# A two-network kernel for one core: the lower weight parts of the first network are added up by DMA instead of subtracted on GpSimd

## The chip, the core and the metric

One core of a Trainium2 chip runs the whole program. The metric is the device time of one execution in microseconds, from the first to the last instruction with what the launch puts around it. The core has five engines that run their own instruction streams and meet only at semaphores: TensorE (PE in the profile; its weight loads are PEld), VectorE (DVE), ScalarE (ACT), GpSimd (POOL) and SyncE (SP, which here only issues DMAs). Sixteen DMA engines move the data of every DMA, whoever issued it.

## What is computed

Three stages on 3072 tokens (4 batches of 768) of width 384 (8 heads of 48):

```
# 1. a complex linear recurrence per head
S_re, S_im = ar * S_re - ai * S_im + kv, ar * S_im + ai * S_re
y[t] = q[t] @ S_re
# 2. the first network (384 -> 1536 -> 384)
xn = x / rms(x) * rms_g
x = (silu(xn @ w_gate) * (xn @ w_val)) @ w_out
# 3. the second network (384 -> 2048 -> 384)
return softplus(x @ w_in) @ w_out2
```

All of it is float32. The large products run in TensorE's faster float32r form, in which an operand keeps fewer bits. So that nothing is lost, each weight w is kept as a pair: an upper part (w rounded to float32r) and a lower part (w minus the upper part). Each product is three matrix products: upper times upper, lower times upper, upper times lower.

## The kernel before

The recurrence is cut into 24 units of 128 tokens (NU). For unit n, VectorE and ScalarE turn the decay factors into packed keys and queries `pk`. SyncE stores `pk` to a scratch in DRAM (`rows_scratch`, L347) and loads it back turned to head rows, `mm` (L340, four DMAs, two for each half of the heads). TensorE then does, for unit m = n - 1 and for each half: transposes of the keys (`kt_of`, L1337), scores (`scores`, L1346), and outputs with the state update (`outputs`, L1357 to L1361). Between them VectorE masks the scores (`mask`, L1026), ScalarE copies the turned keys (`kt_copy`, L610) and the outputs (`y_copy`, L616), and VectorE adds to the state (`state_add`, L1032). TensorE's transposes of the second half wait for the `state_add` of the first, and that one waits for `y_copy`.

The first network works on tiles of 512 tokens, four units each. TensorE's work on tile 0 begins when six units have been prepared (LEAD = 6) and all 36 weight blocks of the first network stand in SBUF. So there is a stretch ahead of tile 0 with steps for units 0, 1 and then a loop of four (`Fori(0, LEAD - 2)`), in which the weights are loaded and split: nine blocks of 128x384 in each step, three groups of three (gate, value, out).

A block passes three engines. SyncE loads it into a staging tile, `stage1[:, kind]`, which lies in `ytile` (`load_w1`, L353). ScalarE copies it into an even slot of `slab`, which rounds it (`w1_hi`, L629, counter `w_hi`). GpSimd subtracts the even slot from the staging tile and writes the odd slot (`w1_lo`, L505, counter `w_lo`). There is one staging tile for each kind, so SyncE loads the next block of a kind only when `w_lo` says that the last one was subtracted.

The order of every engine is written out by hand in its `step`. ScalarE's: the first group of `w1_hi` behind `mid_rest`; then the sums of x, the end roots, `kt_copy` of the first half, and the front of unit n + 1 (`front_sq`, L562, which needs `a_in`; `front_ln`, L566, which needs VectorE's `sum_of`, L839; `front_r0`, L570 and L572; `in_time`, L576); then the second group of `w1_hi`; then `y_copy` of the first half; then the third group, `kt_copy` of the second half, `xh_of` (L623) and `y_copy` of the second half. SyncE's: three loads of weights, the loads of v, `mm` (first half), `a_in` (L325), `mm` (second half), `kq_in` (L329), then six more loads of weights, then the store of `pk`.

At the end of the stretch TensorE waits for `w_hi` and `w_lo` (L1447, L1448) and enters the tiles.

Of the kernel before, what the change touches and what calls it, by code (L numbers as in the profile page):

```python
# [18 lines left out]
F32 = mybir.dt.float32  # L19
F32R = mybir.dt.float32r  # L20
I32 = mybir.dt.int32
ALU = mybir.AluOpType
ACT = mybir.ActivationFunctionType
# [12 lines left out]
F1 = 1536 // P  # L36
# [65 lines left out]
def need(eng, sem, value):  # L102

    if isinstance(value, int) and value <= 0:
        return
    eng.wait_ge(sem, value)


def w2_slot(kind, f):

    if f < F1:
        return 6 * f + 2 * kind
    return 6 * (f - F1 + 4 * kind) + 4
# [16 lines left out]
def program(nc, a_d, kq_d, v_d, w1_d, w2_d, g_d, fa_d, fv_d, out_d):  # L130
    ctx = ExitStack()
    with ctx:
        def sb(name, shape, dt=F32):
            return ctx.enter_context(nc.sbuf_tensor(name, shape, dt))
# [4 lines left out]
        def sem(name):  # L139
            return ctx.enter_context(nc.semaphore(name))  # L140
# [9 lines left out]
        slab = sb("slab", [P, 6 * F1, DM], F32R)  # L150
# [72 lines left out]
        ys_done, y_copied, s_added, decayed = [sem(f"ys_done{i}") for i in range(2)], sem("y_copied"), sem("s_added"), sem("decayed")  # L223
        xt_done, xh_done, xl_done = sem("xt_done"), sem("xh_done"), sem("xl_done")
        w_loaded = [sem(f"w_loaded{i}") for i in range(3)]
        w_hi, w_lo = sem("w_hi"), sem("w_lo")
        w2_loaded = [sem(f"w2_loaded{i}") for i in range(3)]
        w2_hi, w2_lo = sem("w2_hi"), sem("w2_lo")
        gv_done, silu_done, p_done = sem("gv_done"), sem("silu_done"), sem("p_done")
# [26 lines left out]
        stage1 = ytile[:, :, :].rearrange("p a b -> p (a b)")[:, 0:3 * DM].rearrange("p (k n) -> p k n", k=3)  # L256
# [59 lines left out]
        def _(sp):  # L316
            def after(*waits):

                for sem_, value in waits:
                    need(sp, sem_, value)  # L320
# [28 lines left out]
            def load_w1(f):  # L349
                for kind in range(3):  # L350

                    after((w_lo, 3 * f + kind + 1))
                    sp.dma_start(stage1[:, kind, :], w1_d[f, kind]).then_inc(w_loaded[kind], 16)  # L353

            def load_w2(slot):
# [111 lines left out]
        @block.gpsimd  # L467
        def _(pool):
            pool.memset(ident[:, :], 0.0).then_inc(const_gp, 1)
            pool.memset(causal[:, :], 1.0).then_inc(const_gp, 1)  # L470
            pool.memset(state[:, :, :], 0.0).then_inc(const_ready, 1)
            pool.memset(zero[:, :], 0.0).then_inc(const_ready, 1)
            pool.memset(half[:, :], 0.5).then_inc(const_ready, 1)
            pool.memset(eps[:, :], 1e-6).then_inc(const_ready, 1)
            pool.memset(one[:, :], 1.0).then_inc(const_ready, 1)
            pool.memset(tiny[:, :], 1e-22).then_inc(const_ready, 1)
            pool.memset(keep[:, :], 1.0).then_inc(const_gp, 1)
            pool.memset(ok[:, :], 1.0).then_inc(const_ready, 1)
            pool.memset(carry[:, :], 1.0).then_inc(const_ready, 1)
            for buf in (ga, gb):  # L480
                pool.memset(buf[:, 0, :, :], 1.0).then_inc(const_ready, 1)
                pool.memset(buf[:, 1, :, :], 0.0).then_inc(const_ready, 1)
            pool.memset(frame[:, 0, :], 1.0).then_inc(const_ready, 1)
            pool.memset(frame[:, 1, :], 0.0).then_inc(const_ready, 1)
            pool.wait_ge(const_gp, 3)
            pool.affine_select(out=ident[:, :], in_=ident[:, :], compare_op=ALU.not_equal, fill=1.0, base=0,
                               pattern=[[-1, P]], channel_multiplier=1).then_inc(const_ready, 1)

            pool.affine_select(out=causal[:, :], in_=causal[:, :], compare_op=ALU.is_ge, fill=0.0, base=0,
                               pattern=[[1, BK], [BK, NBK]], channel_multiplier=-1).then_inc(const_ready, 1)  # L490

            pool.memset(keep[:, 0::UNITS_B], 0.0).then_inc(const_ready, 1)


            pool.sem_inc(w_lo, 3)

            for counter, start in ((xt_done, 1), (xh_done, 1), (xl_done, 1), (silu_done, 1),
                                   (y_stored, 16), (o_stored, 16)):
                pool.sem_inc(counter, start)

            def w1_lo(f):
                for kind in range(3):
                    pool.wait_ge(w_hi, 3 * f + kind + 1)
                    slot = 6 * f + 2 * kind
                    pool.tensor_tensor(slab[:, slot + 1, :], stage1[:, kind, :], slab[:, slot, :].bitcast(F32),  # L505
                                       ALU.subtract).then_inc(w_lo, 1)

            def w2_lo_of(slot):
                q0 = sum(len(x) for x in W2_PLAN[:slot])
                for i, (kind, f) in enumerate(W2_PLAN[slot]):  # L510
                    at_ = w2_slot(kind, f)
                    pool.wait_ge(w2_hi, q0 + i + 1)
                    pool.tensor_tensor(slab[:, at_ + 1, :], stage2[:, i, :], slab[:, at_, :].bitcast(F32),
                                       ALU.subtract).then_inc(w2_lo, 1)

            def lo(T, f):
                pool.wait_ge(hi_done, F1 * T + f + 3)
                pool.tensor_tensor(pl[:, f % 2, :], hid[:, f % 2, :], ph[:, f % 2, :].bitcast(F32),  # L518
                                   ALU.subtract).then_inc(lo_done, 1)

            def tile(T, last=False):
                for i in range(UT):
                    if last and i:
                        w2_lo_of(3 * i - 1)
                    lo(T, 3 * i)
                    if last:
                        w2_lo_of(3 * i)
                    lo(T, 3 * i + 1)
                    if last:
                        w2_lo_of(3 * i + 1)  # L530
                    lo(T, 3 * i + 2)
                if last:
                    w2_lo_of(F1 - 1)

            with pool.Fori(0, F1) as f:
                w1_lo(f)
            with pool.Fori(0, NT - 1) as T:
                tile(T)
            tile(NT - 1, last=True)

            def lo2(T, f):
                pool.wait_ge(hi2_done, F2 * T + f + 1)
                pool.tensor_tensor(pl[:, f % 2, :], hid[:, f % 2, :], ph[:, f % 2, :].bitcast(F32),  # L543
                                   ALU.subtract).then_inc(lo2_done, 1)

            with pool.Fori(0, NT) as T:
                for f in range(F2):
                    lo2(T, f)
# [3 lines left out]
        def _(act):  # L552
# [73 lines left out]
            def w1_hi(f):  # L626
                for kind in range(3):
                    act.wait_ge(w_loaded[kind], 16 * (f + 1))
                    act.activation(slab[:, 6 * f + 2 * kind, :], stage1[:, kind, :], ACT.Copy).then_inc(w_hi, 1)  # L629

            def w2_hi_of(slot):
                q0 = sum(len(x) for x in W2_PLAN[:slot])
                for i, (kind, f) in enumerate(W2_PLAN[slot]):
                    act.wait_ge(w2_loaded[i], 16 * (sum(1 for q in range(q0) if W2_RANK[q] == i) + 1))

                    act.wait_ge(gv_done, 2 * F1 * (NT - 1) + 2 * slot + 2)
                    if slot >= 2:
                        act.wait_ge(out_done, F1 * (NT - 1) + slot - 2 + 3)
                    act.activation(slab[:, w2_slot(kind, f), :], stage2[:, i, :], ACT.Copy).then_inc(w2_hi, 1)
# [12 lines left out]
            def y_out(T):  # L652
                act.wait_ge(out_done, F1 * T + 2)
                act.wait_ge(y_stored, 16 * (T + 1))
                act.wait_ge(w_lo, 3 * F1 + 3)
                for m in range(2):
                    act.activation(ytile[:, m, :], ybank[m][:, :], ACT.Copy).then_inc(y_act, 1)  # L657

            def step(n, m, x, par=0, col=0, T=None, i=0, w1=None, last=False):
# [7 lines left out]
                if w1 is not None:  # L667
                    w1_hi(w1)
# [25 lines left out]
                if w1 is not None:  # L694
                    w1_hi(w1 + 1)
                if m is not None:
                    y_copy(m, 0)
                if T is not None and i == 0:
                    y_out(T)
                if T is not None:  # L700
                    silu(T, 3 * i + 2)
                if w1 is not None:
                    w1_hi(w1 + 2)
# [123 lines left out]
        def _(dve):  # L827
# [242 lines left out]
            def y_out(T):  # L1070
                dve.wait_ge(out_done, F1 * T + 2)
                dve.wait_ge(y_stored, 16 * (T + 1))
                dve.wait_ge(w_lo, 3 * F1 + 3)
                dve.tensor_copy(ytile[:, 2, :], ybank[2][:, :]).then_inc(y_dve, 1)

            def step(n, m, x, par=0, col=0, T=None, i=0):
# [61 lines left out]
                if T is not None and i == 0:  # L1138
                    y_out(T)
# [185 lines left out]
        def _(pe):  # L1325
# [119 lines left out]
            with pe.Fori(0, LEAD - 2) as k:  # L1445
                step(k + 2, k + 1, k)
            pe.wait_ge(w_hi, 3 * F1)  # L1447
            pe.wait_ge(w_lo, 3 * F1 + 3)  # L1448

            for m in range(NJ):  # L1450
                pe.matmul(ybank[m][:, :], slab[:, 0, 0:P], ph[:, 0, :], start=True, stop=False)
# [143 lines left out]
```

## Time and profile before

| | |
|---|---|
| median of 3 runs | 1201.85 us (1201.65 to 1202.08) |
| time of the profiled execution | 1201.7 us |
| span in its profile, first to last instruction | 1199.9 us |
| around the span | 1.8 us |
| TensorE busy | 1078.1 us, 90% |
| VectorE busy | 725.9 us, 60% |
| ScalarE busy | 665.8 us, 55% |
| GpSimd busy | 295.6 us, 25% |
| GpSimd's 36 subtractions of first-network weights (L505) | 37.1 us, 1051 ns each |
| ScalarE's 36 copies of them (L629) | 17.3 us between 56 and 175 us |
| DMA | 91.22 MB |

Busy shares are means over the whole program. The stretch that the change touches lies between 56 and 175 us; from 175 us on the program is in the tiles.

### The profile page before, as it was taken

The numbers are of one execution on the slowest core, as the hardware profiler recorded it, in microseconds if no ns is written. First come the engines' busy times: TensorE is split into PE (matmuls) and PEld (weight loads), VectorE is DVE, ScalarE is ACT, GpSimd is POOL, SyncE is SP. The second block draws the span as 40 slices with busy tenths as digits, with TensorE's granted clock in tenths as the row PEclk, the third lists the DMA queues.
The fourth block names the chain that finished last, engine by engine and source line by source line (L and its number), as shares of the span: only waits on it lengthen the run. The fifth ranks groups of instructions, "written<-read, shape, count | busy, mean of one in ns | idle before, by whom it ended". The sixth has DMA issues, their size and how long they took to land.

```text
span 1199.9 us, 18970 instructions
## 1 busy us (share of the span) xinstructions
PE 1078.1 (90%) x5495; PEld 915.0 (76%) x5495; DVE 725.9 (60%) x2227; ACT 665.8 (55%) x1184; POOL 295.6 (25%) x260
## 2 busy tenths in 40 slices
PE   0555569999999999999999999989999999999996
PEld 0444468888888788888888878868888888888885
DVE  7799988999999899999999411212221213122211
ACT  3344446566655655565655333456676666676663
POOL 0033331111111111111111115643333333333332
PEclk9999999999999899999999999989999999999999
DMA  1455542443343333334432303320010101010000
GB/s 57 112 147 151 142 140 81 122 120 104 87 113 87 89 87 112 107 100 136 115 88 73 100 1 94 113 97 1 1 53 1 53 1 52 0 52 0 26 1 27
DMA packets 63851, 91.22 MB, mean 76 GB/s; under 512 B 4624, under 2 KB 53648, under 8 KB 63760
## 3 DMA queue, kind: packets, MB, share of 16 engines
q1 hardware_dynamic: 63760, 90.15, 26.4%
q8 instruction: 40, 0.66, 0.2%
q14 instruction: 51, 0.42, 0.1%
HBM read 60.89 MB, written 29.24 MB: 75 GB/s over the span
## 4 chain that ended last, share of the span: by engine, by line
PE 32%; issue 32%; DVE 13%; POOL 10%; DMA 6%; ACT 4%; SPq 1%; DVEq 1%; POOLq 0%; ACTq 0%
PE gbank L1329 14%; POOL pl L543 10%; PE ybank L1329 8%; DVE prep L835 5%; DMA rows_scratch<-pk 3%; PE sbank L1346 3%; DMA mm<-rows_scratch 2%; PE xbank L1358 2%; PE xbank L1357 2%; DVE pk L835 2%; PE xbank L1337 1%; PE xbank L1361 1%; ACT front L562 1%; DVE ga L835 1%; DMA a_in<-in_a 1%
## 5 line engine op out<-in xcount | busy, mean ns | idle before, releaser
L1329 PE MATMUL gbank<-xh,slab 128*128 128x512 f32 x1296 | 406.0, 395 | 3.4 <-issue 2.0
L1329 PE MATMUL ybank<-ph,slab 128*128 128x512 f32 x1020 | 319.6, 395 | 4.9 <-ACT ytile L657 4.0
L1329 PEld LDWEIGHTS gbank<-xh,slab 128*128 128x128 f32 x1296 | 242.5, 190 | 52.8 <-issue 2.1
L1329 PE MATMUL gbank<-xl,slab 128*128 128x512 f32 x648 | 254.0, 392 | 0.0
L1329 PEld LDWEIGHTS ybank<-ph,slab 128*128 128x128 f32 x1020 | 189.3, 189 | 43.2 <-issue 5.7
L518 POOL TENSOR_TENSOR pl<-hid,ph 128x512 fp32r<-128x512 f32 x72 | 98.8, 1372 | 467.6 <-ACT ph L650 467.6
L1329 PE MATMUL ybank<-pl,slab 128*128 128x512 f32 x510 | 199.6, 391 | 0.0
L543 POOL TENSOR_TENSOR pl<-hid,ph 128x512 fp32r<-128x512 f32 x96 | 125.7, 1310 | 268.2 <-ACT ph L772 268.2
L1213 DVE SCALAR_TENSOR_TENSOR hid<-gbank,hid 128x512 f32<-128x512 f32 x72 | 49.7, 691 | 214.5 <-ACT hid L763 214.5
L1329 PEld LDWEIGHTS gbank<-xl,slab 128*128 128x128 f32 x648 | 122.5, 189 | 26.3
L1337 PE MATMUL xbank<-ident,mm 96*128 96x96 f32 x192 | 28.3, 277 | 95.3 <-DMA mm<-rows_scratch 74.5
L1329 PEld LDWEIGHTS ybank<-pl,slab 128*128 128x128 f32 x510 | 96.1, 188 | 20.6
L650 ACT ACTIVATE ph<-hid 128x512 fp32r<-128x512 f32 x72 | 45.9, 637 | 106.8 <-PE ybank L1329 101.4
L1337 PEld LDWEIGHTS xbank<-ident,mm 96*128 96x128 f32 x192 | 20.9, 156 | 107.5 <-issue 102.2
L1067 DVE TENSOR_TENSOR hid<-gbank,hid 128x512 f32<-128x512 f32 x72 | 49.4, 686 | 86.2 <-PE gbank L1329 82.1
L772 ACT ACTIVATE ph<-hid 128x512 fp32r<-128x512 f32 x96 | 60.6, 631 | 72.4 <-DVE hid L1213 70.3
L835 DVE TENSOR_TENSOR prep<-prep 128x384 f32<-128x384 f32 (+2 forms) x264 | 89.5, 368 | 1.7
L1357 PE MATMUL xbank<-v_in,at 128*128 128x48 f32 x384 | 80.7, 296 | 5.3 <-issue 3.3
L1358 PE MATMUL xbank<-state,mm 96*128 96x48 f32 x384 | 83.8, 304 | 0.0
L1357 PEld LDWEIGHTS xbank<-v_in,at 128*128 128x128 f32 x384 | 69.0, 220 | 8.4 <-issue 6.9
L763 ACT ACTIVATE hid<-hid,one 128x512 f32<-128x512 f32 x96 | 69.4, 723 | 3.2
L505 POOL TENSOR_TENSOR slab<-ytile,slab 128x384 f32 x36 | 37.1, 1051 | 130.1 <-ACT slab L629 129.9
(126 smaller groups left out, 1597.1 us busy)
## 6 DMA issues: line engine op xcount, KB each, us to landing
rows_scratch<-pk SPq DMA_DIRECT2D x24, 771.0 KB, 4.9
mm<-rows_scratch SPq DMA_DIRECT2D x96, 192.8 KB, 4.0
a_in<-in_a SPq DMA_DIRECT2D x24, 384.0 KB, 4.7
kq_in<-in_kq SPq DMA_DIRECT2D x24, 384.0 KB, 5.8
ytile<-in_w SPq DMA_DIRECT2D x36, 192.0 KB, 4.7
prep<-in_w SPq DMA_DIRECT2D x32, 192.0 KB, 2.5
y_scratch<-ytile SPq DMA_DIRECT2D x7, 768.0 KB, 5.4
v_in<-in_v SPq DMA_DIRECT2D x24, 192.0 KB, 4.5
```

The costliest lines, as they stand in the source:

```text
L518: pool.tensor_tensor(pl[:, f % 2, :], hid[:, f % 2, :], ph[:, f % 2, :].bitcast(F32), ALU.subtract).then_inc(lo_done, 1)
L543: pool.tensor_tensor(pl[:, f % 2, :], hid[:, f % 2, :], ph[:, f % 2, :].bitcast(F32), ALU.subtract).then_inc(lo2_done, 1)
L650: act.activation(ph[:, f % 2, :], hid[:, f % 2, :], ACT.Copy).then_inc(hi_done, 1)
L763: act.activation(hid[:, f % 2, :], hid[:, f % 2, :], ACT.Ln, bias=one[:, 0:1]).then_inc(l_done, 1)
L772: act.activation(ph[:, f % 2, :], hid[:, f % 2, :], ACT.Copy).then_inc(hi2_done, 1)
L835: tick(dve.tensor_tensor(out, a, b, op))
L1067: dve.tensor_tensor(hid[:, f % 2, :], gbank[(2 * f + 1) % 3][:, :], hid[:, f % 2, :], ALU.mult).then_inc(p_done, 1)
L1213: dve.scalar_tensor_tensor(out=hid[:, f % 2, :], in0=hbank[f % 4][:, :], scalar=0.0, in1=hid[:, f % 2, :], op0=ALU.max, op1=ALU.add).then_ ...
L1329: last = pe.matmul(out, slab[:, slot + part, cols], x, start=f, stop=l)
L1337: last = pe.transpose(xbank[:, h * 2 * D:(h + 1) * 2 * D], mm[:, hf * HH + h, 0:CH], ident[0:2 * D, 0:2 * D])
L1357: pe.matmul(xbank[:, h * D:(h + 1) * D], at[:, h, :], v_in[:, head, :], start=True, stop=False)
L1358: pe.matmul(xbank[:, h * D:(h + 1) * D], mm[:, head, CH:2 * CH], state[:, head, :], start=False, stop=True)
```

## The change

ScalarE, having written the upper part into the even slot, waits for its own write and then writes the negative of it into the odd slot (counter `w_neg`). GpSimd no longer computes: it waits for `w_neg` and issues a DMA that reads the block a second time from DRAM and adds it onto the odd slot, which gives w minus the upper part there. Its completion counts on `w_lo`, now by 16 for each block. SyncE's loads and the two `y_out` now wait for `w_neg` in place of `w_lo`, since only ScalarE reads the staging tile. TensorE's entry to the tiles waits for all 36 adding DMAs, and once more on `silu_done`, which has been counted up long before. GpSimd's loop over the twelve groups is written out.

```diff
             def load_w1(f):
                 for kind in range(3):
-                    after((w_lo, 3 * f + kind + 1))
+                    after((w_neg, 3 * f + kind + 1))
                     sp.dma_start(stage1[:, kind, :], w1_d[f, kind]).then_inc(w_loaded[kind], 16)
...
-            pool.sem_inc(w_lo, 3)
+            pool.sem_inc(w_neg, 3)
...
             def w1_lo(f):
                 for kind in range(3):
-                    pool.wait_ge(w_hi, 3 * f + kind + 1)
-                    slot = 6 * f + 2 * kind
-                    pool.tensor_tensor(slab[:, slot + 1, :], stage1[:, kind, :], slab[:, slot, :].bitcast(F32),
-                                       ALU.subtract).then_inc(w_lo, 1)
+                    pool.wait_ge(w_neg, 3 * f + kind + 4)
+                    pool.dma_start(slab[:, 6 * f + 2 * kind + 1, :], w1_d[f, kind],
+                                   accum_op=ALU.add).then_inc(w_lo, 16)
...
-            with pool.Fori(0, F1) as f:
+            for f in range(F1):
                 w1_lo(f)
...
                     act.activation(slab[:, 6 * f + 2 * kind, :], stage1[:, kind, :], ACT.Copy).then_inc(w_hi, 1)
+                    act.wait_ge(w_hi, 3 * f + kind + 1)
+                    act.activation(slab[:, 6 * f + 2 * kind + 1, :], slab[:, 6 * f + 2 * kind, :].bitcast(F32), ACT.Copy,
+                                   scale=-1.0).then_inc(w_neg, 1)
...
-                act.wait_ge(w_lo, 3 * F1 + 3)
+                act.wait_ge(w_neg, 3 * F1 + 3)
...
-                dve.wait_ge(w_lo, 3 * F1 + 3)
+                dve.wait_ge(w_neg, 3 * F1 + 3)
...
             pe.wait_ge(w_hi, 3 * F1)
-            pe.wait_ge(w_lo, 3 * F1 + 3)
+            pe.wait_ge(w_lo, 16 * 3 * F1)
+            pe.wait_ge(silu_done, 1)
```

ScalarE, in the loop of four steps, the first group of weight copies and what stands behind it, before (`slab<-ytile` is the upper part, `xn,xs<-xnat` the sums of x):

```order
L629 ISA [waits w_loaded0]
L629 ACTIVATE slab<-ytile 128x384
L629 ISA [waits w_loaded1]
L629 ACTIVATE slab<-ytile 128x384
L629 ISA [waits w_loaded2]
L629 ACTIVATE slab<-ytile 128x384
L106 ISA
L601 ACTIVATE xn,xs<-xnat 128x384 [waits xt_done,y_copied]
```

The same place in the changed kernel, where the lines above the function are numbered one lower (`slab<-slab` is the negative):

```order
L628 ISA [waits w_loaded0]
L628 ACTIVATE slab<-ytile 128x384
L629 ISA
L630 ISA [waits w_hi]
L630 ACTIVATE slab<-slab 128x384
L628 ISA [waits w_loaded1]
L628 ACTIVATE slab<-ytile 128x384
L629 REGISTER_ALU
L630 ISA [waits w_hi]
L630 ACTIVATE slab<-slab 128x384
```

Each copy is followed by a wait for itself and a second activation of the same size, and all that stood behind the three copies stands behind six activations; the same holds for the second and third group.

GpSimd, from the last constant on, before:

```order
L492 MEMSET keep 128x5
L535 UNCONDITIONAL_BRANCH
L535 ISA
L505 ISA [waits w_hi]
L505 ISA x2
L505 TENSOR_TENSOR slab<-ytile,slab 128x384
```

And in the changed kernel, up to the first instruction of the tiles:

```order
L492 MEMSET keep 128x5
L504 DMA slab<-in_w 128x384 [waits w_neg] x36
L536 UNCONDITIONAL_BRANCH
L536 ISA
L517 ISA
L517 TENSOR_TENSOR pl<-hid,ph 128x512 [waits hi_done]
```

The twelve rounds of three subtractions have become 36 issues of DMAs, and nothing computes on GpSimd ahead of the tiles. SyncE's order is the same in both kernels; only the counter that its loads wait for is another.

## Rows read from the trace of the kernel before

**Rows 1.** Busy time by stretch: us; engines with instructions; clock; DMA share; GB/s.
```profile
90.00:120.00 30.00, 15.62 (x75) 14.80 (x75) 28.08 (x86) 13.42 (x30) 9.15 (x9) 1.00 0.54 151
175.00:700.00 525.00, 516.06 (x3001) 441.70 (x3001) 468.38 (x1586) 295.66 (x550) 79.06 (x57) 0.99 0.36 100
```

**Rows 2.** The chain that ended last, 0 to 200 us: start us, us, what.
```profile
114.93 5.51 DMA rows_scratch<-pk
...
120.83 3.73 DMA mm<-rows_scratch
...
144.72 5.67 DMA rows_scratch<-pk
...
175.42 1.41 PE ybank L1451 x3
```

**Rows 3.** VectorE in time order, step n = 3: start us, us, idle before it.
```profile
97.67 0.69 DVE L1026 TENSOR_TENSOR at<-sbank,causal 128x512 f32<-128x512 f32 x1 [1.34 <-PE sbank L1346]
...
98.97 0.55 DVE L839 TENSOR_TENSOR front<-front 128x384 f32<-128x384 f32 x1
...
102.98 0.96 DVE L835 TENSOR_TENSOR scaled<-frame,gv 128x6 f32<-128x6 f32 x1
...
103.97 1.98 DVE L835 TENSOR_TENSOR prep<-ga,scaled 128x96 f32<-128x96 f32 x2
...
106.24 0.34 DVE L1032 TENSOR_TENSOR state<-xbank,state 96x192 f32<-96x192 f32 x1
...
109.70 0.68 DVE L1026 TENSOR_TENSOR at<-sbank,causal 128x512 f32<-128x512 f32 x1
```

**Rows 4.** GpSimd in time order, the second group of that step.
```profile
102.74 3.09 POOL L505 TENSOR_TENSOR slab<-ytile,slab 128x384 f32 x3 [7.67 <-ACT slab L629]
```

**Rows 5.** VectorE in time order, step n = 1, which has no weights.
```profile
46.31 0.16 DVE L835 TENSOR_TENSOR scaled<-frame,gv 128x6 f32<-128x6 f32 x1
...
46.50 0.43 DVE L835 TENSOR_TENSOR prep<-ga,scaled 128x96 f32<-128x96 f32 x2
...
47.83 0.35 DVE L1032 TENSOR_TENSOR state<-xbank,state 96x192 f32<-96x192 f32 x1 [0.54 <-ACT xnat L616]
...
51.00 0.69 DVE L1026 TENSOR_TENSOR at<-sbank,causal 128x512 f32<-128x512 f32 x1 [1.12 <-PE sbank L1346]
```

**Rows 6.** ScalarE in time order, step n = 3.
```profile
97.07 0.84 ACT L562 ACTIVATE front<-a_in 128x768 f32<-128x768 f32 x1
...
100.20 0.52 ACT L570 ACTIVATE front<-front 128x384 f32<-128x384 f32 x1
100.75 0.52 ACT L572 ACTIVATE front<-front 128x384 f32<-128x384 f32 x1
...
101.86 1.34 ACT L629 ACTIVATE slab<-ytile 128x384 f32 x3
103.48 0.33 ACT L616 ACTIVATE xnat<-xbank 128x192 f32<-128x192 f32 x1 [0.27 <-PE xbank L1361]
```

**Rows 7.** DMA issues by SyncE in that step, in time order: start us, us, what.
```profile
92.03 0.36 SPq L325 DMA_DIRECT2D a_in<-in_a  x1
...
94.14 12.20 SPq L353 DMA_DIRECT2D ytile<-in_w  x6
```

**Rows 8.** From issue to landing: `a_in` (L325), then the first three weight loads.
```profile
DMA to landing us min/median/max: 4.3/4.3/4.3
...
DMA to landing us min/median/max: 5.1/5.2/5.3
```

**Rows 9.** The same step by single microseconds; columns as in the first group.
```profile
96.00:97.00 1.00, 1.00 (x7) 1.00 (x6) 0.32 (x2) 1.00 (x2) 0.00 (x0) 1.00 1.13 196
...
98.00:99.00 1.00, 0.54 (x3) 0.57 (x3) 1.00 (x7) 0.01 (x1) 0.00 (x0) 1.00 1.05 384
...
102.00:103.00 1.00, 1.00 (x9) 1.00 (x8) 0.90 (x8) 1.00 (x4) 0.26 (x1) 1.00 0.00 0
```

**Rows 10.** ScalarE in time order, the last weight copy of the program.
```profile
168.16 0.52 ACT L629 ACTIVATE slab<-ytile 128x384 f32 x1 [0.66 <-DMA ytile<-in_w]
```

More of the change, by code:

```diff
@@ L225, in program @@
         w_loaded = [sem(f"w_loaded{i}") for i in range(3)]
-        w_hi, w_lo = sem("w_hi"), sem("w_lo")
+        w_hi, w_neg, w_lo = sem("w_hi"), sem("w_neg"), sem("w_lo")
         w2_loaded = [sem(f"w2_loaded{i}") for i in range(3)]
```

## The prediction

> **What bounds the kernel now.** I read the busy time by stretch first. From 175 us on TensorE is busy 516.06 of 525 us [rows 1], so whatever moves TensorE's entry into the tiles moves the end by about as much. Between 90 and 120 us it is another picture: TensorE 15.62 of 30 us, VectorE 28.08 of 30, DMA 0.54 [rows 1]. The chain of waits says what paces this stretch: a step's store of `pk` starts at 114.93, the next at 144.72, a period of 29.8 us. In between come 5.51 us of store, then the load of `mm`, landing 3.73 us after 120.83 [rows 2], TensorE's scores, VectorE's mask, and from the mask on VectorE alone until its `pk` is ready. Entry to the tiles is at 175.42 [rows 2]; TensorE finds the weights ready then.
>
> The first half of a step ends in a wait for this round trip of DMAs: VectorE sat idle 1.34 us before its mask at 97.67 [rows 3]. What is saved there becomes more idle time. Only the half behind the mask counts: from 97.67 to `state_add` at 106.24, to the second mask at 109.70, to the store at 114.93 [rows 2, 3].
>
> **What goes: GpSimd's subtractions.** In that half GpSimd computes from 102.74 on for 3.09 us [rows 4]. VectorE's `scaled` takes 0.96 us there and the two products behind it 1.98 [rows 3]. The same instructions in the step without weights take 0.16 and 0.43 us [rows 5]. So the subtractions hold VectorE back by 0.80 + 1.55 = 2.35 us before `state_add`; without them VectorE would be there at 106.24 - 2.35 = 103.89.
>
> The Trainium skill (SBUF — State Buffer, Who interferes with whom) says that a VectorE instruction with two SBUF inputs contends with a GpSimd instruction that reads SBUF, and not with one that only writes. The trace agrees with the first half, by 0.96 against 0.16 us; the second half, which would let the new DMA issues pass without harm to VectorE, no row of before shows.
>
> **What comes on ScalarE.** Three negatives behind each group's copies. Dependent activations of this size start 0.55 us apart (100.20 and 100.75); independent ones (1.34 - 0.52)/2 = 0.41 us apart [rows 6]. A copy with its negative costs 0.55 + 0.41 = 0.96 us, a group 2.88 instead of 1.34. The first group's extra 1.5 us lies before `kt_copy`, for which ScalarE waits on the `mm` round trip anyway; with that cover gone it would cost up to 1.5 us a step. The second group stands right ahead of `y_copy`, for which VectorE's `state_add` and then TensorE's transposes wait. Starting at 101.86 as now, the group would end at 104.74, `y_copy` takes 0.33 [rows 6], and `state_add` follows at about 105.15. ScalarE therefore takes back 1.25 of the 2.35 us, and the gain there is at most 106.24 - 105.15 = 1.1 us. The third group ends ahead of need: SyncE's next loads are let go by ScalarE instead of GpSimd, about as early as before.
>
> **What comes on the DMA engines.** Nine more transfers of 192 KB a step, which read the weights once more from DRAM, read the slab, and write it. Their cost c, in time of all 16 engines, has no row. From below: the bytes moved once at the fastest rate seen, 197 kB at 384 GB/s, 0.5 us. From above: twice the bytes at the slow rate of the head-row loads, 2 x 197 kB at 196 GB/s, 2.0 us [rows 9]. The nearest row is the plain load of the same block, also about 0.5 us (a landing each half microsecond at the end of the first three loads, below), and an add reads twice as much: I take c = 1.1, with a little for the second descriptor.
>
> The Trainium skill puts the reason in the same way (Collectives: The Full Stack, The bandwidth ceiling): an add in a DMA reads two sources, and the throughput measured there falls from 62.28 to 32.35 GB/s, by 1.93. By that estimate c would be 0.5 x 1.93 = 1.0, and the sum below 1 us lower.
>
> Where do they fall? The first group's negatives end at about 92.4, 93.3 and 94.3; allowing some 1.8 us for GpSimd's issue and the start (an estimate from the way of SyncE's DMAs, whose traffic starts about a microsecond behind the issue), the adds move from 94.2 on. There the DMA engines are full: shares 1.13 and 1.05 at 96 and 98 us, none at 102 [rows 9]. Every engine-microsecond of adds pushes something back:
> - `a_in`, issued at 92.03, lands 4.3 us later, 96.3 [rows 7, 8]. Its last 1.4 us of traffic run at half rate or worse, landing 97.7 to 99. ScalarE takes it at 97.07 [rows 6]; VectorE needs the squares 0.95 us later, at 98.97 [rows 3]. Until 98.0 that costs nothing; beyond, up to 1 us. I take nothing.
> - The three loads for the second group: issued from 94.14 to 95.3, landing 5.1 to 5.3 us later [rows 7, 8], at 99.4 to 100.4. Behind three adds they land 3c = 3.3 us later, the first at 102.7, and now this ends ScalarE's wait, not the 101.86 of before. Second group 102.75 to 105.65, `y_copy` to 106.0, `state_add` 106.05: a gain of 0.2.
>
> The Trainium skill (DMA: Bandwidth & Descriptors, Issuing engines are not separate DMA queues) says that spreading DMAs over issuing engines gives no bandwidth, since all run on the same 16 engines. Only SyncE issues data DMAs in this trace, so no row shows it. Were GpSimd's queue a path of its own, the 3.3 us would not arise and the cheap case below would hold.
>
> **Behind `state_add`.** The second mask stands 109.70 - 106.24 = 3.46 us behind it [rows 3] and 51.00 - 47.83 = 3.17 in the step without weights, where it waits for TensorE [rows 5]. So of GpSimd's delay in this part only 0.3 us come off; the rest turns into waiting for scores. Behind the second mask I count nothing: GpSimd is nearly done by then. Per step 0.2 + 0.3 = 0.5 us, for four steps 2.0 us.
>
> **The entry.** The last copy is at 168.16 [rows 10], its negative done at 169.2. An adding DMA with 3 to 4 us from there to landing is in at 173, before TensorE's 175.42 - 2.0 = 173.4. Nothing for it, but the cover is thin. `silu_done`, the `w_neg` waits of `y_out` and the unrolled loop wait for what is long past: nothing.
>
> **The sum.** 1201.7 (profiled execution) - 2.0 = 1199.7; that execution stands 0.15 under the median of 1201.85. Forecast 1199.8, a change of 0.17%.
>
> **Rivals.**
> - *The adds are cheap or fall beside the traffic* (c near 0.5, or started so late that the loads pass first). Then `state_add` is at ScalarE's bound: 1.1 + 0.3 = 1.4 us a step, 5.6 in all, 1196.2. For it: the idle stretch from 100 us on. Against: the full shares before it.
> - *The adds are dear, slower than before.* Place: the loads for the second group, behind the first group's adds. The time of `state_add` is 99.4 + 3c + 3.3; with the 0.3 us behind it, it breaks even at c = 1.26, and a measurable loss begins above c = 1.45. At c = 2.0 the loads come at most 5.5 us later, as they get half the engines at worst: 105.0, `state_add` 108.2, 1.65 us a step, 6.6 in all, 1208.3. Against it only the reasoning on bytes.
> - *The last adds land late and TensorE waits at its entry.* Decides from the point where the last add takes over 4.2 us behind its negative. If GpSimd needed 3 us for each issue, the three of the last group would end at about 176 and land at 178: 4.6 us of wait on top of the 2.0 gained, 1204.3. The Trainium skill has a rule for such a delay (SBUF — State Buffer, Who interferes with whom): GpSimd cannot write its descriptors while VectorE runs an instruction in a mode that takes both ports. Few of VectorE's here could be of that kind; no row shows it.
> - *The change does less than it says*: GpSimd's issuing holds VectorE up as the subtractions did. Then the 0.3 goes too and little is left: 1201.5, inside the forecast's range.
>
> **Chances.** Forecast and the last rival 0.37 (1197.5 to 1203.5), cheap 0.28, dear 0.22, late 0.13. The range 1195.8 to 1208.0 leaves out the deep ends. A measurement of this kernel can tell 0.2%, 2.4 us: faster than 1199.45 is the cheap case and part of the forecast's own, 0.38; slower is the dear case and most of the late one, 0.31; the rest 0.31.
>
> **What would show it.** Right: no GpSimd computing before 175 us; `scaled` at 0.16 us in the loop; a period near 29.3 us; ScalarE waiting for weight loads at 102.7, not starting at 101.9; DMA landings of `a_in` and the second group's loads 1.5 to 3.3 us longer; entry at about 173.4 with no wait for a DMA. Wrong: landings as before (cheap), or loads landing beyond 104 and a period over 30 us (dear), or a DMA as releaser of the first `ybank` product (late); a wait for `a_in` that moves VectorE's `sum_of` would break the step in which I took nothing.

## The result and the profile after

The changed kernel takes 1206.6 us (median of 4 runs, 1205.76 to 1207.57), beside 1201.75 us for the kernel before on the same chip: a ratio of 1.0047, with a 95% interval of 1.0034 to 1.0059. (The two medians alone divide to 1.0040, inside that interval.) It is 5 us slower. 1199.8 was forecast, 0.17% faster; the time lies inside the range, on the other side of no change.

The profiled execution has a span of 1204.0 us, 4.1 more than before. The page shows the new traffic as a queue of its own:

```profile
span 1204.0 us, 18931 instructions
...
q1 hardware_dynamic: 63760, 90.15, 26.4%
q0 software_dynamic: 5184, 7.08, 3.7%
```

Busy time by stretch, as in [rows 1]:

```profile
90.00:120.00 30.00, 15.96 (x75) 14.77 (x75) 21.56 (x85) 17.83 (x40) 7.67 (x9) 1.00 0.87 204
175.00:700.00 525.00, 514.34 (x3000) 440.79 (x3001) 470.94 (x1590) 295.79 (x551) 80.08 (x58) 1.00 0.37 101
```

VectorE is busy 21.56 us of 30 where it was 28.08, ScalarE 17.83 where it was 13.42, the DMA engines 0.87 where they were 0.54. So VectorE is freed as announced, and the stretch is none the shorter for it. SyncE's and TensorE's timelines give the stores of `pk` and the entry, the entry of the kernel before last:

```profile
85.42 0.39 SPq L347 DMA_DIRECT2D rows_scratch<-pk  x1
115.64 0.38 SPq L347 DMA_DIRECT2D rows_scratch<-pk  x1
146.48 0.38 SPq L347 DMA_DIRECT2D rows_scratch<-pk  x1
178.44 0.38 SPq L347 DMA_DIRECT2D rows_scratch<-pk  x1
```
```profile
180.26 1.63 PE L1454 MATMUL ybank<-ph,slab 128*128 128x512 f32 x3
```
```profile
175.21 1.63 PE L1451 MATMUL ybank<-ph,slab 128*128 128x512 f32 x3
```

(The chain in [rows 2] puts that entry at 175.42; all entries below are read from the timelines.) From the first store of the loop at 55.16 the mean period is 30.82 us, beside 29.69 before (55.70 to 174.47), and TensorE enters the tiles at 180.26 instead of 175.21. The whole loss, 5.05 us at the entry and 4.1 in the span, arises ahead of the tiles.

VectorE in the same step as [rows 3], start, length and the idle time before:

```profile
97.92 0.69 DVE L1028 TENSOR_TENSOR at<-sbank,causal 128x512 f32<-128x512 f32 x1 [1.73 <-PE sbank L1348]
...
103.23 0.15 DVE L837 TENSOR_TENSOR scaled<-frame,gv 128x6 f32<-128x6 f32 x1
...
105.89 0.35 DVE L1034 TENSOR_TENSOR state<-xbank,state 96x192 f32<-96x192 f32 x1 [1.67 <-ACT xnat L615]
...
109.06 0.69 DVE L1028 TENSOR_TENSOR at<-sbank,causal 128x512 f32<-128x512 f32 x1 [1.12 <-PE sbank L1348]
...
113.18 0.56 DVE L1063 TENSOR_TENSOR xl<-sbank,xh 128x384 f32 x1 [1.45 <-ACT xh L622]
```

`scaled` is at 0.15 us. `state_add` comes 7.97 us behind the first mask, 8.57 before, and the second mask 3.17 behind that, 3.46 before: together 0.9 us gained in this step, against 0.5 in the sum. But it is the second of four steps that differ. From the first mask to `state_add` they take 7.77, 7.97, 9.10 and 9.24 us, in the mean 8.52, where each took 8.57 or 8.58 before; the mean gain is 0.35 us a step. In the last two steps ScalarE waits for the second group's loads, 1.13 and 1.27 us. Behind the second mask stands a wait that was not there, 1.45 us for ScalarE's `xh_of`. ScalarE shows why:

```profile
106.00 0.52 ACT L628 ACTIVATE slab<-ytile 128x384 f32 x1
106.66 0.52 ACT L630 ACTIVATE slab<-slab  x1
109.04 0.52 ACT L628 ACTIVATE slab<-ytile 128x384 f32 x1 [1.86 <-DMA ytile<-in_w]
109.70 0.53 ACT L630 ACTIVATE slab<-slab  x1
111.08 0.52 ACT L628 ACTIVATE slab<-ytile 128x384 f32 x1 [0.86 <-DMA ytile<-in_w]
111.74 0.52 ACT L630 ACTIVATE slab<-slab  x1
112.17 0.47 ACT L609 ACTIVATE kt<-xbank 128x384 f32<-128x384 f32 x1
112.54 0.48 ACT L622 ACTIVATE xh<-sbank 128x384 f32 x1
```

This is the third group. Its loads were issued from 103.6 to 105.8, as before (104.08 to 106.0); how long they took to land is, first before, then after:

```profile
DMA to landing us min/median/max: 2.4/2.6/2.6
```
```profile
DMA to landing us min/median/max: 2.3/4.2/5.2
```

`kt_copy` and `xh_of` stand behind the group. At the end of the last step it is worse: the last load is taken at 173.88, `kt_copy` at 174.96 instead of 168.59, and TensorE waits for it there. Over the stretch TensorE waited 8.7 us in four times for `kt_copy` and VectorE 6.1 us in four times for `xh_of`; before, neither had such a wait.

### The profile page after: what moved, and what is told of

It is laid out like the page before. It is cut to its first block, busy times and chain, and to the rows that moved or that the text cites. A ratio compares the mean times of both kernels' runs of the same rounds, so it can differ in the third digit from the quotient of the medians.

```text
span 1204.0 us, 18931 instructions
## 1 busy us (share of the span) xinstructions
PE 1077.1 (89%) x5495; PEld 912.6 (76%) x5495; DVE 702.7 (58%) x2227; ACT 684.5 (57%) x1220; POOL 289.4 (24%) x260
## 4 chain that ended last, share of the span: by engine, by line
PE 31%; issue 30%; DMA 11%; DVE 10%; POOL 10%; ACT 5%; SPq 1%; DVEq 0%; POOLq 0%; ACTq 0%
PE gbank L1331 14%; POOL pl L542 10%; PE ybank L1331 8%; DMA rows_scratch<-pk 4%; DVE prep L837 3%; DMA ytile<-in_w 3%; PE sbank L1348 2%; DMA mm<-rows_scratch 2%; PE xbank L1360 2%; PE xbank L1359 2%; DVE pk L837 2%; PE xbank L1363 1%; DMA a_in<-in_a 1%; PE xbank L1339 1%; ACT front L561 1%
## 5 line engine op out<-in xcount | busy, mean ns | idle before, releaser
L1360 PEld LDWEIGHTS xbank<-state,mm 96*128 96x128 f32 x384 | 68.0, 221 | 0.0
```

The costliest lines, as they stand in the source:

```text
L1360: pe.matmul(xbank[:, h * D:(h + 1) * D], mm[:, head, CH:2 * CH], state[:, head, :], start=False, stop=True)
```

## The experiments

Ratios are to the kernel before on the same chip, with the 95% interval. The period is the mean of the four from the store at about 55 us on; the entry is the start of TensorE's first `ybank` product. Period and entry come from the one profiled execution of a run. That execution is 1.9 us longer than the run's median in e6 and 3.7 us longer in e10, so these two periods and entries are too long. The runs were made on more than one chip; a difference of two ratios is uncertain by about 0.2%.

| run | ratio | interval | period, us | entry, us |
|---|---|---|---|---|
| before | 1 | | 29.69 | 175.21 |
| changed | 1.0047 | 1.0034 to 1.0059 | 30.82 | 180.26 |
| e1 no adds | 0.9958 | 0.9944 to 0.9973 | 28.74 | 170.67 |
| e2 no subtractions | 0.9944 | 0.9925 to 0.9964 | 27.29 | 169.66 |
| e3 plain loads | 0.9995 | 0.9981 to 1.0008 | 29.76 | 176.46 |
| e4 third group late | 1.0105 | 1.0085 to 1.0125 | 30.82 | 186.71 |
| e5 adds of group 1 | 0.9978 | 0.9964 to 0.9992 | 29.11 | 172.58 |
| e6 adds of group 2 | 1.0023 | 1.0012 to 1.0035 | 30.66 | 180.24 |
| e7 adds of group 3 | 0.9961 | 0.9947 to 0.9974 | 28.65 | 170.57 |
| e8 mixed | 0.9953 | 0.9936 to 0.9970 | 29.31 | 170.88 |
| e9 hold group 2 | 1.0070 | 1.0044 to 1.0096 | 31.40 | 182.24 |
| e10 negatives late | 1.0044 | 1.0029 to 1.0060 | 31.50 | 182.79 |
| e11 mixed, held | 0.9935 | 0.9922 to 0.9949 | 28.61 | 168.32 |

The timelines of VectorE and SyncE split the period into four parts, here in us, as means of the four steps:

| run | store of `pk` to first mask | to `state_add` | to second mask | to next store |
|---|---|---|---|---|
| before | 12.43 | 8.58 | 3.46 | 5.23 |
| changed | 12.46 | 8.52 | 3.17 | 6.67 |
| e1 no adds | 12.75 | 7.77 | 3.17 | 5.05 |
| e5 adds of group 1 | 12.70 | 8.19 | 3.17 | 5.05 |
| e6 adds of group 2 | 12.77 | 7.77 | 3.17 | 6.95 |
| e9 hold group 2 | 14.83 | 7.96 | 3.17 | 5.44 |
| e11 mixed, held | 13.04 | 6.23 | 3.16 | 6.18 |

### The three parts of the change: e1, e2, e3

e1 takes the adding DMAs out of the changed kernel:

```diff
-                    pool.dma_start(slab[:, 6 * f + 2 * kind + 1, :], w1_d[f, kind],
-                                   accum_op=ALU.add).then_inc(w_lo, 16)
+                    pool.sem_inc(w_lo, 16)
```

> The changed kernel without the 36 adding DMAs: GpSimd waits for the negative and only counts it as done, so the odd slots hold the negatives and the lower parts are missing from the result. ScalarE's 36 negatives and all waits stay. Theory A (the adds' traffic delays the weight loads, and ScalarE's kt_copy and xh_of stand behind the third group of them): the loads land as before, VectorE's waits for xh_of go, and the gain that was forecast for cheap adds appears: 1196 to 1198 us. Theory B (the 36 activations and their waits on ScalarE are the cost): 1205 to 1207 us, as the changed kernel.

0.9958, that is 5.0 us faster than before; the expectation's 1196 to 1198 us were 0.995 to 0.997 of 1201.75. All that stays of the change, without its traffic, brings what the cheap rival promised (5.6 us). VectorE's waits for `xh_of` and TensorE's for `kt_copy` are gone. Theory B, that ScalarE's activations are the loss, falls.

e2 takes the subtractions out of the kernel before:

```diff
+            pool.memset(slab[:, 1::2, :].bitcast(F32), 0.0).then_inc(w_lo, 3)
-            pool.sem_inc(w_lo, 3)
...
-                    slot = 6 * f + 2 * kind
-                    pool.tensor_tensor(slab[:, slot + 1, :], stage1[:, kind, :], slab[:, slot, :].bitcast(F32),
-                                       ALU.subtract).then_inc(w_lo, 1)
+                    pool.sem_inc(w_lo, 1)
```

> The kernel before without GpSimd's 36 subtractions: it only counts; the odd slots are set to zero once at the start, so the lower weight parts are missing from the result. Both theories: this shows what the subtractions cost VectorE, about 2.35 us before state_add and 0.3 behind it per step, so 2.6 us x 4 = 10 us at most: 1191 to 1193 us. If VectorE's longer instructions in that stretch were not due to GpSimd, 1201.8 us as before.

The period falls from 29.69 to 27.29, 2.40 a step, nearly the 2.6 expected. The ratio, 0.9944, shows only 6.7 us of it, because clearing the slots cost some 4 us at the start (the store before the loop is at 59.57, before at 55.70), told below. The periods give ScalarE's part too: 28.74 with negatives and without adds, 27.29 without both, so the negatives take back 1.45 us a step; 1.25 were forecast.

e3 keeps the DMAs but not the adding:

```diff
-                    pool.dma_start(slab[:, 6 * f + 2 * kind + 1, :], w1_d[f, kind],
-                                   accum_op=ALU.add).then_inc(w_lo, 16)
+                    pool.dma_start(slab[:, 6 * f + 2 * kind + 1, :], w1_d[f, kind]).then_inc(w_lo, 16)
```

> The changed kernel with a plain load in place of each add (same issuer, same source, same destination, same number; it overwrites the negative, so the odd slots hold the full weights). It leaves out the read of the slab in the DMA. Theory A with the price in the second read: an add measured about 1.24 us of all engines, a plain load should take about 0.5 to 0.6, so most of the delay goes: 1198 to 1201 us. Theory A with the price in any extra transfer from a second queue, add or not: 1204 to 1207 us. Theory B: 1205 to 1207 us.

0.9995, between the two theories. From e1 on, the plain transfers cost 0.37% and adding costs another 0.52%, each give or take 0.2%. So neither the second read nor the mere number of transfers is the whole price. In the stretch GpSimd's queue took, by its share of the DMA engines,

```profile
q0 software_dynamic: 5022, 6.87, 36.2%
```

of 119 us (56 to 175 us of the changed kernel) for 35 adds, 1.23 us of all engines for each. With plain loads it was 25.0% of 110 us for 6.64 MB, or 34 transfers, 0.81 us each. Both shares contain some waiting for the other queue, so they are ends from above.

### Which adds cost: e5, e6, e7

Each keeps the adds of one group of every step, here the first, and leaves out the others:

```diff
+                    if f % 3 == 0:
                         pool.dma_start(slab[:, 6 * f + 2 * kind + 1, :], w1_d[f, kind],
                                        accum_op=ALU.add).then_inc(w_lo, 16)
...
-            pe.wait_ge(w_lo, 16 * 3 * F1)
+            pe.wait_ge(w_lo, 16 * F1)
+            pe.wait_ge(w_neg, 3 * F1 + 3)
```

> The changed kernel with adding DMAs for the first group of each step only (12 of 36); the others are left out, so their lower parts are missing from the result. Measured against the kernel before on the same chip; no adds at all gave a ratio of 0.9958 and all 36 adds 1.0047, a difference of 0.9% or 11 us. Theory of placement: the first group's adds run beside mm, a_in and the second group's loads while the DMA engines are full, and alone give back half of it: ratio 0.999 to 1.001. Theory of load alone (each add costs the same wherever it falls): a third, ratio 0.9985 to 0.9990.

> The same with adds for the second group only. They fall between 105 and 109 us of a step, beside the third group's loads, behind which kt_copy and xh_of stand. Theory of placement: 1 to 1.5 us a step where the third group's slack is used up, ratio 0.9975 to 0.9995. Theory of load alone: 0.9985 to 0.9990.

> The same with adds for the third group only. They fall beside nothing but the next step's store of pk. Theory of placement: next to no cost, ratio 0.9955 to 0.9970. Theory of load alone: 0.9985 to 0.9990.

Above e1's 0.9958 the first group costs 0.20%, the second 0.65%, the third 0.03%. The sum is 0.88%, and all three together cost 0.89% (1.0047 - 0.9958), so the parts add up, as far as intervals of about 0.14% on each ratio let one say; the first group's part is barely clear of nothing, the third's is not. The theory of load alone, a third each, falls by e6 and e7. The placement theory holds, but I had put the dear place at the first group, and it is the second: e5 and e6 both missed their numbers, one below and one above. In e6 the third group's loads are taken as late as in the changed kernel, and `kt_copy` with them:

```profile
108.04 0.52 ACT L629 ACTIVATE slab<-ytile 128x384 f32 x1 [0.23 <-DMA ytile<-in_w]
110.82 0.52 ACT L629 ACTIVATE slab<-ytile 128x384 f32 x1 [1.60 <-DMA ytile<-in_w]
113.47 0.52 ACT L629 ACTIVATE slab<-ytile 128x384 f32 x1 [1.46 <-DMA ytile<-in_w]
114.55 0.47 ACT L610 ACTIVATE kt<-xbank 128x384 f32<-128x384 f32 x1
```

and its entry, 180.24 in a long execution, comes near that of the changed kernel, 180.26. In the table of parts its whole loss stands behind the second mask, 6.95 against 5.05 us. In e5 and e7 neither the wait for `xh_of` nor the one for `kt_copy` exists.

### Moving the price away: e4, e9, e10

e4 lets `kt_copy` and `xh_of` pass ahead of the third group on ScalarE:

```diff
-                if w1 is not None:
-                    w1_hi(w1 + 2)
                 if m is not None:
                     kt_copy(m, 1)
...
                     xh_of(x, par, col, T)
+                if w1 is not None:
+                    w1_hi(w1 + 2)
```

> The changed kernel with one move on ScalarE: kt_copy of the second half and xh_of stand ahead of the third group of weight copies instead of behind it. Traffic and activations stay the same. Theory A in its sharp form (the delayed loads hurt only through what stands behind the third group): VectorE's wait for xh_of, 1.45 to 2.2 us a step, goes: 1199 to 1202 us. If the loss sat elsewhere (slower mm, a_in or pk transfers): 1205 to 1207 us. The price of the move: the third group ends later, and with it the last adds, so TensorE may wait at its entry.

1.0105, far worse, a miss of every number written down. VectorE's wait for `xh_of` did go. But the third group's adds now fall on the store of `pk`, which takes 8.0 us to land instead of 5.7, and VectorE waits 15.9 us in four times for `mm`, where the changed kernel had 4.7. TensorE then waits 6.74 us at its entry, right behind the last adds:

```profile
186.71 1.62 PE L1454 MATMUL ybank<-ph,slab 128*128 128x512 f32 x3 [6.74 <-issue]
```

That is the third rival of the prediction, brought about by the move. The profile names no DMA as its releaser, but the last add is issued at 179.53 and takes 7.1 us to land, thus until 186.6.

e9 keeps the order and holds back only the second group's adds:

```diff
             for f in range(F1):
+                if f in (1, 4, 7):
+                    pool.wait_ge(w_neg, 3 * (f + 1) + 6)
                 w1_lo(f)
```

> The changed kernel, complete, with one more wait on GpSimd: in the first three steps it issues the second group's adds only when the third group's last negative is written, thus when the third group's weight loads have landed; in the last step nothing changes. Same traffic, other time. If the second group's adds cost 0.65% because they delay the third group's loads, three quarters of that, 0.5%, comes back: ratio 0.9995 to 1.001 against the kernel before, where the changed kernel had 1.0047. If the amount of traffic counts and not its place (it then falls on the next step's store of pk and load of mm): 1.003 to 1.006.

1.0070, a miss again; the interval overlaps that of the changed kernel. In the first three steps the third group is on time: `kt_copy` is at 110.69, and VectorE's wait for `xh_of` is 1.5 us, once, in the last step. But six adds now run right before and beside the store of `pk`. How long the store takes from issue to landing, changed kernel first, then e9:

```profile
DMA to landing us min/median/max: 5.7/5.7/5.7
```
```profile
DMA to landing us min/median/max: 8.6/8.6/8.6
```

With the `mm` loads behind it, VectorE's wait for them is 16.8 us in four times. Half of my theory stands (the second group's adds are what delays the third group's loads), and half falls (that they could be put elsewhere in the step for nothing). Nine adds of 1.23 us and the traffic of before, 52.7% of 119 us or 15.7 us a step, make 27 us of a period of 30, which leaves little room for them to go unnoticed.

e10 puts the three negatives of the second group behind `y_copy`:

```diff
                 if w1 is not None:
-                    w1_hi(w1 + 1)
+                    w1_hi(w1 + 1, late=True)
                 if m is not None:
                     y_copy(m, 0)
+                if w1 is not None:
+                    for kind in range(3):
+                        neg(w1 + 1, kind)
```

> The changed kernel, complete, with the second group's three negatives on ScalarE behind y_copy instead of ahead of it. If ScalarE's place ahead of y_copy costs 1.1 to 1.4 us a step (its wait shown as VectorE's state_add waiting 1.45 us for it without adds): ratio 0.999 to 1.002. If the late weight loads set the time of the group anyway and the third group then ends later: 1.003 to 1.006.

1.0044, no change. VectorE's wait for `y_copy` falls from 11.4 to 4.8 us over the stretch, and its wait for `xh_of` rises from 6.1 to 14.2; as this trace is of the long execution, the second number shows where the time went more than how much it was. The time gained ahead of the third group is lost behind it, as the second expectation had it.

### A kernel that beats both: e8, e11

The second group's subtractions are the dear ones for VectorE (the 2.35 us). So e8 leaves the first and third group to GpSimd, takes the second by negatives and adds, and puts its negatives behind `y_copy`. As nothing is subtracted from the staging tiles of the second group, SyncE's loads of the third wait only for the second's copies (`w_hi`):

```diff
+                    if f % 3 == 1:
+                        pool.wait_ge(w_neg, f - f // 3 * 3 + 3 * (f // 3) - 1 + kind + 1)
+                        pool.dma_start(slab[:, slot + 1, :], w1_d[f, kind], accum_op=ALU.add).then_inc(w_add, 16)
+                        continue
                     pool.wait_ge(w_hi, 3 * f + kind + 1)
...
                     w1_hi(w1 + 1)
                 if m is not None:
                     y_copy(m, 0)
+                if w1 is not None:
+                    w1_neg(w1 + 1)
...
+            pe.wait_ge(w_add, 16 * F1)
```

> A whole kernel with the full result: GpSimd subtracts the first and third group as before, and only the second group, whose subtractions held VectorE back by 2.35 us a step, goes by negatives and adding DMAs; on ScalarE the three negatives stand behind y_copy instead of ahead of it. If the losses were understood (traffic of 3 adds a step beside the third group's loads, 1 us a step; VectorE freed, 2.35 + 0.3 us a step): 4 to 7 us faster than the kernel before, ratio 0.994 to 0.997. If the third group's subtractions hold VectorE once the second group's are gone, or any use of adding DMAs costs what it brings: 0.999 to 1.001.

0.9953, as expected. e11 issues those adds behind the third group's subtractions, except in the last step:

```diff
-            for f in range(F1):
+            for f in (0, 2, 1, 3, 5, 4, 6, 8, 7, 9, 10, 11):
                 w1_lo(f)
```

> The mixed kernel, complete (first and third group subtracted by GpSimd, second by negatives and adds), with the second group's adds issued behind the third group's subtractions in the first three steps. If the mixed kernel's adds delay the third group's loads as in the changed kernel, up to three quarters of 0.65% comes off its 0.9953: ratio 0.990 to 0.993. If in it GpSimd's subtractions of the third group are the bound, 0.995 to 0.997.

0.9935, 7.8 us faster by the ratio than the kernel before (the medians are 1194.15 and 1201.56 us), with a period of 28.61. This misses 0.990 to 0.993 by a little. The intervals of e8 and e11 overlap, so only the gain of each over the kernel before is shown, not that of e11 over e8. VectorE in e11:

```profile
96.41 0.69 DVE L1041 TENSOR_TENSOR at<-sbank,causal 128x512 f32<-128x512 f32 x1 [1.73 <-PE sbank L1361]
...
101.74 0.15 DVE L850 TENSOR_TENSOR scaled<-frame,gv 128x6 f32<-128x6 f32 x1
101.93 0.43 DVE L850 TENSOR_TENSOR prep<-ga,scaled 128x96 f32<-128x96 f32 x2
102.64 0.35 DVE L1047 TENSOR_TENSOR state<-xbank,state 96x192 f32<-96x192 f32 x1
105.81 0.69 DVE L1041 TENSOR_TENSOR at<-sbank,causal 128x512 f32<-128x512 f32 x1 [1.12 <-PE sbank L1361]
106.42 2.87 DVE L850 TENSOR_TENSOR prep<-prep 128x96 f32<-128x96 f32 x5
```

`state_add` comes 6.23 us behind the mask and does not wait for ScalarE: the full 2.35 us are there. What is left to gain stands behind the second mask. The five products at 106.42 take 2.87 us beside GpSimd's subtractions of the third group (104.46 to 107.52), and 2.07 us in e1, where nothing is subtracted. So the third group's subtractions are not free either: about 0.8 us a step.

## Why the prediction was wrong

By its own steps:

- **What goes.** Right. `scaled` is at 0.15 us, the two products at 0.43. Behind `state_add` 0.3 us came off, as said. Prediction and expectation together put 2.6 us a step on the subtractions as the most there is; e2 measures 2.40.
- **ScalarE.** Right in place, a little short in size: 1.25 us a step forecast, 1.45 measured (e1 against e2). VectorE waits 1.46 us for `y_copy` in e1. A copy with its negative takes 1.07 us (92.52 to 93.59), where the prediction had 0.96.
- **The price of an add.** c = 1.1 was taken; the share gives 1.23, an end from above. The bounds held, and the dear rival's point of 1.26 was not passed.
- **The first group's adds.** The mechanism is there: the second group's loads take 7.7 to 8.3 us instead of 5.1 to 5.3 [rows 8], 2.6 to 3.0 more where 3.3 was forecast. `a_in` takes 4.8 instead of 4.3 us, and `sum_of` was not moved in this step. The forecast counted this as 1.4 - 0.5 = 0.9 us a step, 3.6 in all. In the changed kernel `state_add` is 0.75 us a step later than without adds (8.52 against 7.77), 3.0 in all; e5 gives 0.20%, 2.4 us.
- **The step that failed: "The third group ends ahead of need".** I looked only at when the loads are let go, which did not change, and not at what they meet; and I counted nothing behind the second mask, where `xh_of` is needed. The second group's adds are issued from 103.7 to 105.9 and run beside exactly these loads, in a stretch that I had read as idle. In the changed kernel the part behind the second mask is 1.62 us a step longer than without adds (6.67 against 5.05), 6.5 us in all; e6 puts the term at 0.65%, 7.8 us. The sum has nothing for it. Part by part, the forecast was -5.6 without traffic, +3.6 for the first group's adds and nothing for the others, -2.0; the runs give -5.0 (e1), +2.4 (e5), +7.8 (e6) and +0.4 (e7), +5.6, which is the ratio 1.0047.
- **The third group's adds.** Nothing was counted; 0.03% was measured, which is nothing within the noise.
- **The entry.** No wait for the adds appeared, as forecast: the last is issued at 175.35 and lands 3.7 us later, at 179.1, before 180.26. The entry is late because `kt_copy` is, which stands behind the same loads.
- **The rule on issuing engines.** By the Trainium skill (DMA: Bandwidth & Descriptors, Issuing engines are not separate DMA queues) GpSimd's transfers interleave with SyncE's on the same 16 engines. The trace agrees: loads of the same 192 KB take 4.2 us (median of the third group) beside GpSimd's transfers and 2.6 us without.
- **Small sums.** The last rival's 1201.5 does not follow from its terms: without the 0.3 us, 0.2 a step is left, 0.8 in all, thus 1201.0. With c = 1.0 the sum would be 1.2 us lower, not 1. Neither changes the forecast.

Of the rivals the dear one comes nearest, in sign and with three quarters of its size at c = 2.0 (5 us lost instead of 6.6), but its condition and its place did not come true: c is no more than 1.23, below its break-even of 1.26, and the loads that decide are the third group's. They are late at a smaller c as well: in e3, where a transfer costs at most 0.81 us, TensorE still waits 4.5 us for `kt_copy` and VectorE 1.9 us for `xh_of`. That the time fell inside the range is luck: a loss on a path not looked at, of the size of those that were.

## What to carry to other kernels

A transfer that replaces an instruction must be laid against the transfers that run at its time, group by group, and a gap in the DMA share is no room if a load on the chain is issued into it a microsecond later. Where the same operation is repeated, look for the repetition that costs: here 12 of 36 subtractions held the chain back most and 12 of 36 adds did most of the harm, and replacing only those 12, at another place in ScalarE's order, beat both kernels. One step is not the loop: the step read first had 0.9 us of gain, the mean of the four 0.35. On an engine with a fixed order, ask of each wait what stands behind it; moving one piece out of the way (e4, e9, e10) moved the wait to the next.

## What the runs showed of the hardware

An add from GpSimd's queue costs clearly more than a plain transfer of the same block: 1.23 against 0.81 us of all engines by the shares, each 192 KB in rows of 1536 bytes; in the whole time 36 plain transfers cost 0.37% and their adding another 0.52%. Issuing an add occupied GpSimd for 0.84 to 0.86 us (a plain transfer 0.53 in e3), a little less than the subtraction of such a block takes (1.05 us), but without holding VectorE. In e9 VectorE's five products behind the second mask (110.98 to 113.05) take 2.07 us beside GpSimd's issues, which run from 111.08 on; in e1, without any, they take the same. Two issues of the changed kernel:

```profile
92.91 0.86 POOL L504 DMA_DIRECT2D slab<-in_w  x1 [9.73 <-ACT slab L630]
93.98 0.84 POOL L504 DMA_DIRECT2D slab<-in_w  x1 [0.21 <-issue]
```

The other surprise is in e2. GpSimd's clearing of the slots only writes SBUF, yet one VectorE instruction waited for it. First e2, GpSimd's clearing and two instructions of VectorE, then the second of them in the kernel before:

```profile
2.94 11.61 POOL L495 MEMSET slab<- 128x13824 f32 x1
...
9.28 0.56 DVE L846 SCALAR_TENSOR_TENSOR front<-front 128x384 f32<-128x384 f32 x1
...
9.89 4.88 DVE L851 TENSOR_SCALAR front<-front 128x384 f32<-128x384 f32 x1
```
```profile
10.22 0.36 DVE L853 TENSOR_SCALAR front<-front 128x384 f32<-128x384 f32 x1
```

4.88 us instead of 0.36, until the clearing ended at 14.55, while the instruction with two SBUF inputs at 9.28 took its usual 0.56. By the Trainium skill (SBUF — State Buffer, Who interferes with whom), VectorE's `tensor_scalar` can run in a mode that takes both ports and then waits for any GpSimd instruction, and one with two SBUF inputs waits only for a GpSimd instruction that reads; the trace agrees in both halves. It is why e2's ratio understates the subtractions.
